# Order of the last two tiles in the second feed-forward phase of a one-core attention and MLP kernel

## The reference

```python
def _attn_ref(q, k, v):                      # q, k, v: (4, 8, 768, 64)
    for t in range(S):
        state = gamma * state + outer(k[t], v[t])
        y[t] = scale * q[t] @ state

def _moe_ref(x, w_in, w_out):                # x: (3072, 512), d_ff 2048
    h = x @ w_in
    g = np.where(h >= 1, h, np.where(h <= -1, 0.0, (h + 1) ** 2 / 4))
    return g @ w_out

def _moe2_ref(x, w_in, w_out, g_ln):         # x: (3072, 512), d_ff 1024
    h = x @ w_in
    e = np.exp(h - h.max(-1))
    solu = h * e / (e.sum(-1) + 1e-09)
    ln = (solu - solu.mean(-1)) / np.sqrt(solu.var(-1) + 1e-6) * g_ln
    return ln @ w_out
```

## Time and profile before

| what | value |
|---|---|
| median of 3 runs | 891.05 us (891.0 to 892.11) |
| the profiled execution's own time | 890.45 us |
| its span, first to last instruction | 888.7 us |
| TensorE matmul busy | 873.4 us, 98% of the span |
| VectorE, ScalarE, GpSimd busy | 411.9, 283.0 and 211.6 us |

### The profile page before, as it was taken

How to read it: one execution, slowest core, us unless ns; L and a number is a source line. 1 busy time by engine, 2 the same in 40 slices (tenths; PEclk the granted TensorE clock), 3 DMA queues, 4 the chain that set the end, 5 groups by cost and what they waited for, 6 DMA issues and landing times.

```text
span 888.7 us, 11899 instructions
## 1 busy us (share of the span) xinstructions
PE 873.4 (98%) x4864; PEld 719.5 (81%) x4864; DVE 411.9 (46%) x666; ACT 283.0 (32%) x438; POOL 211.6 (24%) x185
## 2 busy tenths in 40 slices
PE   6999999999999999999999999999999999999997
PEld 5788888888888888888888888888888888888886
DVE  5544443333433343333433343443566666666662
ACT  2333342122312232122322133334334444444442
POOL 2555432223222323223222112226100000000000
PEclk9999999999999999999999999999999999999999
DMA  9912102111111111211101104300444444444443
GB/s 347 340 49 69 63 4 92 48 48 48 48 60 48 48 36 66 76 50 36 48 36 36 36 1 166 119 1 0 143 131 146 156 149 142 145 152 150 158 133 104
DMA packets 50742, 82.84 MB, mean 93 GB/s; under 512 B 5248, under 2 KB 23680, under 8 KB 50688
## 3 DMA queue, kind: packets, MB, share of 16 engines
q1 hardware_dynamic: 50400, 81.56, 27.0%
q10 hardware_dynamic: 288, 0.53, 0.2%
HBM read 56.90 MB, written 25.17 MB: 92 GB/s over the span
## 4 chain that ended last, share of the span: by engine, by line
PE 67%; DVE 18%; issue 5%; ACT 4%; DMA 3%; POOL 2%; SPq 1%; POOLq 0%; ACTq 0%; DVEq 0%
PE acc L342 30%; PE h L329 29%; DVE solu L804 3%; DVE zq L819 3%; ACT e L755 3%; DVE h_max L794 3%; DVE zT_lo L785 3%; PE att L270 2%; PE att L283 2%; DVE z L815 2%; PE att L286 2%; POOL rstd L832 1%; DVE x_lo L777 1%; DMA mask<-in_mask 1%; PE att L299 1%
## 5 line engine op out<-in xcount | busy, mean ns | idle before, releaser
L342 PE MATMUL acc<-g_hi,w 128*128 128x512 f32 x768 | 256.8, 395 | 0.0
L329 PE MATMUL h<-x_hi,w 128*128 128x512 f32 x768 | 252.4, 390 | 3.6 <-DVE x_lo L458 2.1
L608 POOL TENSOR_TENSOR g_lo<-g_raw,g_hi 128x512 fp32r<-128x512 f32 x96 | 123.4, 1285 | 404.5 <-ACT g_hi L369 404.5
L418 ACT ACTIVATE g_raw<-g_raw,half_bias 128x512 f32<-128x512 f32 x96 | 69.5, 724 | 347.6 <-DVE g_raw L543 347.6
L329 PEld LDWEIGHTS h<-x_hi,w 128*128 128x128 f32 x768 | 144.2, 188 | 34.0 <-ACT x_hi L369 2.4
L342 PEld LDWEIGHTS acc<-g_hi,w 128*128 128x128 f32 x768 | 144.1, 188 | 33.1 <-issue 0.7
L543 DVE TENSOR_SCALAR g_raw<-h 128x512 f32<-128x512 f32 x96 | 66.4, 691 | 185.1 <-PE acc L342 184.3
L342 PE MATMUL acc<-g_lo,w 128*128 128x512 f32 x384 | 149.8, 390 | 0.0
L329 PE MATMUL h<-x_lo,w 128*128 128x512 f32 x384 | 149.4, 389 | 0.0
L548 DVE TENSOR_TENSOR g_raw<-h,g_raw 128x512 f32<-128x512 f32 x96 | 66.4, 692 | 62.3 <-ACT g_raw L418 61.7
L329 PEld LDWEIGHTS h<-x_lo,w 128*128 128x128 f32 x384 | 72.1, 188 | 14.9
(11 more groups left out here) (69 smaller groups left out, 872.6 us busy)
## 6 DMA issues: line engine op xcount, KB each, us to landing
z<-zq SPq DMA_DIRECT2D x24, 512.0 KB, 2.6
zt<-z SPq DMA_DIRECT2D x96, 128.0 KB, 2.9
kT<-in_kT SPq DMA_DIRECT2D x24, 256.0 KB, 2.7
q<-in_q SPq DMA_DIRECT2D x24, 256.0 KB, 2.7
v<-in_v SPq DMA_DIRECT2D x24, 256.0 KB, 2.9
x2T<-y SPq DMA_DIRECT2D x24, 256.0 KB, 2.6
x_raw<-x2T SPq DMA_DIRECT2D x12, 512.0 KB, 4.3
out<-o SPq DMA_DIRECT2D x24, 256.0 KB, 2.0
```

The lines of the kernel that those rows point to most:

```text
L329: last = mm(hb[f % 2][:, :], ww, xx[:, kt, :], start=kt == 0 and t == 0, stop=kt == KT - 1 and t == 2)
L342: last = mm(acc[m][:, :], ww, gg[:, f % 2, :], start=f == 0 and t == 0, stop=f == FT1 - 1 and t == 2)
L418: nc.scalar.activation(gate[:, f % 2, :], gate[:, f % 2, :], ACT.Square, bias=half_bias[:, 0:1], scale=0.5).then_inc(sem["squared"], 1)
L608: tt(g[1][:, f % 2, :], gate[:, f % 2, :], g[0][:, f % 2, :].bitcast(F32), ALU.subtract)\
```

## The change

The loops over t end two tiles early on ScalarE and VectorE, and the rest is written out. The helper functions `exponential`, `squares` (ScalarE) and `maximum`, `softened`, `normalized` (VectorE) hold the instructions that stood in the loop bodies, unchanged. On TensorE up(23) moves ahead of down(19); five down products follow. SyncE stores tiles 19 to 23 after the last turn. GpSimd's list is as it was.

```diff
@@ SyncE
             for t in range(TILES):
                 if t % 2 and t // 2 + 2 < TILES // 2:
                     load_x2(t // 2 + 2)
-                if t >= LAG2:
+                if LAG2 <= t < TILES - 2:
                     store(t - LAG2)
                 turn(t)
-            for t in range(TILES - LAG2, TILES):
+            for t in range(TILES - 2 - LAG2, TILES):
                 store(t)
@@ ScalarE, after the loop (now range(TILES - 2))
-            output(TILES - 3)
+            exponential(TILES - 2)
+            squares(TILES - 2)
+            exponential(TILES - 1)
+            split_z(TILES - 3)
+            squares(TILES - 1)
+            output(TILES - 5)
+            split_z(TILES - 2)
+            output(TILES - 4)
             split_z(TILES - 1)
-            output(TILES - 2)
-            output(TILES - 1)
+            for t in range(TILES - 3, TILES):
+                output(t)
@@ VectorE, after the loop (now range(TILES - 2))
+            maximum(TILES - 2)
+            softened(TILES - 2)
+            maximum(TILES - 1)
+            normalized(TILES - 2)
+            softened(TILES - 1)
+            split_z(TILES - 3)
+            normalized(TILES - 1)
+            split_z(TILES - 2)
             split_z(TILES - 1)
```

More of the change, by code:

```diff
@@ L748, in output, with exponential @@
                 copy(o[:, t % 2, :], op[t % 2][:, :]).then_inc(sem["o_ready"], 1)
-            for t in range(TILES):
-                if t >= 2 and t % 2 == 0 and t // 2 + 1 < TILES // 2:
-                    split_x(t // 2 + 1)
+            def exponential(t):
                 act.wait_ge(sem["neg_max"], t + 1)
@@ L756, in _, with squares @@
                                      accum_out=st("e_sum", t)).then_inc(sem["e_ready"], 1)
+            def squares(t):
                 act.wait_ge(sem["neg_mean"], t + 1)
@@ L759, in _ @@
                                      accum_out=st("sq_sum", t)).then_inc(sem["sq_sum"], 1)
+            for t in range(TILES - 2):
+                if t >= 2 and t % 2 == 0 and t // 2 + 1 < TILES // 2:
+                    split_x(t // 2 + 1)
+                exponential(t)
+                squares(t)
                 if t == 0:
@@ L786, in split_z, with maximum @@
                         .then_inc(sem["zT_lo"], 1)
[L788 to L792, removed]
+            def maximum(t):
                 dve.wait_ge(sem["h2_ready"], 2 * t + 2)
-                nc.vector.tensor_reduce(st("h_max", t), h, AX.X, ALU.max).then_inc(sem["h_max"], 1)
+                nc.vector.tensor_reduce(st("h_max", t), hp[t % 2][:, :], AX.X, ALU.max).then_inc(sem["h_max"], 1)
                 dve.wait_ge(sem["h_max"], t + 1)
@@ L797, in _, with softened @@
                     .then_inc(sem["neg_max"], 1)
+            def softened(t):
                 dve.wait_ge(sem["e_ready"], t + 1)
@@ L803, in _ @@
                 dve.wait_ge(sem["e_inv"], t + 1)
-                nc.vector.scalar_tensor_tensor(solu[:, :], e[:, :], st("e_inv", t), h, ALU.mult, ALU.mult,
-                                               accum_out=st("s_sum", t)).then_inc(sem["h2_used"], 1)
+                nc.vector.scalar_tensor_tensor(solu[:, :], e[:, :], st("e_inv", t), hp[t % 2][:, :], ALU.mult,
+                                               ALU.mult, accum_out=st("s_sum", t)).then_inc(sem["h2_used"], 1)
                 dve.wait_ge(sem["h2_used"], t + 1)
@@ L808, in _, with normalized @@
                     .then_inc(sem["neg_mean"], 1)
-                if t == 0:
-                    finish["dve_evacuate"]()
+            def normalized(t):
                 dve.wait_ge(sem["sq_sum"], t + 1)
@@ L821, in _ @@
                     .then_inc(sem["zq_ready"], 1)
+            dve.wait_ge(sem["power_set"], 1)
+            for t in range(TILES - 2):
+                if t >= 2 and t % 2 == 0 and t // 2 + 1 < TILES // 2:
+                    split_x(t // 2 + 1)
+                maximum(t)
+                softened(t)
+                if t == 0:
+                    finish["dve_evacuate"]()
+                normalized(t)
                 if t:
                     split_z(t - 1)
+            maximum(TILES - 2)
[6 more added lines that the diff above has]
+            split_z(TILES - 2)
             split_z(TILES - 1)
```

## The result

| | before | after |
|---|---|---|
| median | 891.15 us (12 runs, 889.83 to 892.38) | 888.95 us (12 runs, 887.95 to 889.56) |
| ratio | | 0.9976, 95% interval 0.9967 to 0.9985 |
| profiled execution | 890.45, span 888.7 | 889.20, span 887.4 |

The change is faster: 2.2 us between the medians, 1.3 to 2.9 us by the interval. The forecast was 889.3 us and 1.75 us less, which lies inside the interval.

What follows compares the result with a forecast made beforehand. TensorE was taken to set the pace, with one stop ahead of down(23). The stop's 1.62 us plus 0.13 us slow start make 1.75 us less: 891.05 - 1.75 = 889.3 us, range 888.7 to 890.4.

Steps and rivals of the forecast that it cites:

- The stop, 1.62 us: TensorE's only wait over the last tiles, ahead of down(23), released by `zT_lo`; forecast to vanish, gaining 1.62 us.
- the slow start: down(23) takes 5.34 us to its last start where its steps make 5.21; forecast to save another 0.13 us.
- The layout with the old durations: New order timed with the old profile's durations: tile 23's `zq` ends at 867.5, some 3.7 us earlier.
- the time to spare: Slack ahead of down(23), wanted at 878.16: about 2.0 us for its turned data, 1.8 us for output(21).
- What could be late next: Margins of data for down(21) to down(23): closest output(21), ending at 876.4, wanted at 878.16, 1.8 us left.
- the second rival: The stop only moves, ahead of down(21) or down(22): about 891.0 us, chance 4%.
- The round trips: Stores and loads back of tiles 22 and 23, now 6.1 us apart instead of 9.9; overlap taken to cost nothing.
- the rival of a part gain: Round trips of tiles 22 and 23 get in each other's way: gain only 0.7 us, 890.3 us, chance 7%.
- its 2.9 us: Upper estimate of the growth of tile 23's store and last load together from overlap: 1.7 + 1.2 us.
- the 2.0 us of `zT`: Spare time ahead of down(23): its data ready at 876.1, TensorE there at 878.16.
- The rival on the slower side: down(23) hangs on output(21), that on store(19): over 0.2% slower from a 9.1 us store landing, chance 2%.
- within 0.2%: Outcome of no change told apart, 0.2% being 1.78 us: 53%, against 45% faster and 2% slower.

Runs made afterwards that it cites:

- e2: The changed kernel, measured a second time: 888.71 us, ratio 0.9977 to the kernel before.
- e7: The changed kernel with tile 23's transposes on VectorE done twice, with a wait between: 888.39 us, ratio 0.9966 to the kernel before.
- e8: The changed kernel with tile 23's transposes on VectorE done four times, with waits: 891.81 us, ratio 1.001 to the kernel before.
- e9: As e6, but with output(19) moved ahead of exponential(23) on ScalarE: 890.80 us, ratio 1.0 to the kernel before.
- e6: The changed kernel with VectorE and ScalarE back to tile 22 and then tile 23, output copies left as changed: 890.42 us, ratio 1.0003 to before.
- e3: The changed kernel with TensorE alone back in its old order, down(19) between up(22) and up(23): 892.87 us, ratio 1.0025 to the kernel before.
- e4: The changed kernel with SyncE's part alone undone, store(19) ahead of turn(22) and store(20) ahead of turn(23): 896.77 us, ratio 1.007 to before.
- e5: TensorE in the new order, with VectorE, ScalarE and SyncE in the order of the kernel before: 893.21 us, ratio 1.0026 to the kernel before.
- e10: The kernel before with tile 23's transposes done twice: 892.83 us, ratio 1.0021 to the kernel before.
- e1: The kernel before, unchanged, measured a second time: 890.34 us, ratio 0.9995.
- e11: The kernel before, unchanged, run for one more profile: 890.66 us.
- e12: The kernel before, unchanged, run again for one more profile: 890.31 us.

## Why the prediction was right

**The stop, 1.62 us, was the gain.** Right. It was there in all four profiles of before (1.62, 1.52, 1.57, 1.39 us) and in none of the change. The first profile had the longest of the four, so the sum was 0.1 us high there. At equal clock the change is worth 1.5 to 1.9 us. The 0.13 us for the slow start is gone in the profile of after too, but is too small to be told apart in the times.

**The layout with the old durations.** Its times on VectorE, ScalarE and SyncE were met to 0.25 us. Tile 23's maximum: laid out for 857.1, found at 857.30; its `var` 864.6 against 864.66; `zq` ending 867.5 against 867.57; loads from 870.1 against 870.23; output(21) 875.8 against 875.80. So close a match is partly luck. In this execution tile 22's maximum started 0.33 us later than before (852.84 against 852.51), and the new list then took 0.35 us less than laid out: 23.54 us from there to the end of output(21), where 23.89 were laid out. That, and not only the 0.50 us by which TensorE was late, is why the time to spare came out as 2.3 us and not 1.8. It was 2.28 us in e2, 2.1 in e7, which started 0.5 us earlier than before, and 2.2 by e8.

**What could be late next.** output(21) was named as the closest, and it is what stops TensorE in e8 and e9. output(19), laid out to end at 865.2 for a product at 867.28, had 2.1 us to spare; e6 shows that it stops TensorE as soon as squares(23) is late. So the second rival, a stop that only moves ahead of down(21), is what the change would have been in e6's order. Closer than any of these was the maximum of tile 23: up(23)'s last matmul ends at 856.67 + 0.39 = 857.06 and the maximum starts at 857.30, 0.24 us apart where the layout had 0.5, since TensorE was late.

**The round trips.** I took nothing for their overlap, against an estimate of 3.6 us from the Trainium skill ("DMA: Bandwidth & Descriptors", "Latency and other measured facts", 2 us of HBM access at high load). The trace shows 2.64 and 4.52 us for tile 23's two legs, within 0.04 us of before; no such growth came, and the rival of a part gain falls. That rival also had a slip: it set its 2.9 us against the 2.0 us of `zT`, but the same loads feed output(21), which had 1.8 us, so by its own numbers down(23) would have started 1.1 us late and the gain would have been 0.5 us, not 0.7.

**The rival on the slower side** (down(23) hangs on output(21), that on store(19)) is a real dependence, and e8 shows output(21) releasing the stop; store(19) itself never was late. A slower outcome by leaving a part out is easy, as e3, e4 and e5 show; the change has all of them.

**The size.** The medians moved 2.2 us (e2: 1.8), I said 1.75; the interval 1.3 to 2.9 holds it. Part of the 2.2 is the sample: the twelve executions of before beside the change have a median of 891.15, the 76 beside the experiments 890.58, and after's 888.95 is 1.6 us below that. I put 53% on "within 0.2%", 45% on faster by more; at 0.24% it fell on the other side of that border, and the interval of 0.15 to 0.33% holds the border too. What the forecast had as plain scatter of the runs, 891.05 against the profiled 890.45, is in part TensorE's clock: 42 of before's 76 executions had a mean below 1.000, and the 34 of them at 0.998 are 1.0 us slower in the median. The share that the stop has in it stays open: a mean of 0.996 or less appeared in before, e3, e4, e5, e6, e8 and e10, which all have a stop, and in none of the 33 executions of after, e2 and e7, which have none; but before had it only in 5 of 76, and e1 and e9, which have the stop too, in none of 21, so this is no proof for the kernel before. Two executions of before at 0.998 took 894.56 and 895.00 us, over 4 us above those at 1.000; neither kind of fall costs that much in a profile, and the cause of these two is open.

## What to carry to other kernels

- At the end of a software pipeline the steady order is no longer the best: with no more input to prepare, the serial steps of the last two tiles can be laid into each other's waits, if the matrix product that feeds the last tile is moved forward. Lay the new order out with the durations of the old profile; here the time to spare came out 0.3 to 0.5 us larger than laid out.
- Such a reordering is a set. A product moved later drags its output copy, the copy drags its store, and a store that waits in SyncE's list holds the loads behind it (e4). Leaving out TensorE's part, SyncE's or the interleaving made it as slow as before or slower (0 to +6 us).
- Sort the executions by granted clock before reading differences below 0.3%.

## What the runs showed of the hardware

A stop can cost more than its length, since TensorE's clock can fall behind it. In the profiles with an idle time of 2.12 (e5), 2.20 (e10), 2.38 (e3) and 3.68 us (e4) ahead of a product, the granted clock was at the lower level behind it (0.50 in a slice of 2 us of e3), and the starts of matmuls were 0.43 us apart for a time (about 3.5 us in e5 and e10), which cost 1.6 to 1.8 us. In the nine stops with 0.99 to 1.53 us idle (before, e1, e11, e12, e6, e8, e9 and the first stops of e4 and e5) it stayed at 1.00. So e10's stop of 2.36 us cost 4.0 us, and e8's of 1.63 us only itself and 0.13. It is not so in every execution: five of e5's nine had a mean clock of 1.000. The Trainium skill, "TensorE: Matmul & The Clock Gate", section "Wait — 56ns, not 53.3ns?", gives 426.7 ns from start to start for 512 columns at the lower clock, and the trace agrees with 0.43 us; for the upper clock it gives 215.7 ns, where this kernel, with a weight load for each matmul, shows 226.7.

The clock also falls in the first 30 us in part of the executions, where TensorE works between waits (it is busy for 76 and 85% of the two slices above). Seven of the fourteen profiles show it (0.98 and 0.85 of full clock in after, 0.93 and 0.90 in e2, and the like in e4, e5, e8, e9 and e10), none of them of the kernel before unchanged. In these, down(1) starts 0.5 to 1.2 us later than in the first profile of before; in the six others beside it, from 0.5 us earlier to 0.3 us later.
